# Scores of a fused attention kernel made four tiles ahead in one step, and what moves with them on VectorE and GpSimd

## The chip, the cores and the metric

The kernel runs on one core of a Trainium2 chip. The metric is device time in microseconds (us) of one execution. A core has five engines, each with its own list of instructions that it works through in order: TensorE (PE, matmuls; its weight loads are shown as PEld), VectorE (DVE), ScalarE (ACT), GpSimd (POOL) and SyncE (SP, which issues DMAs). They wait for one another by semaphores only.

## The reference

Three stages follow one another: attention that keeps the 32 largest scores of each row, a mixture of experts with a routing that runs along the sequence, and a Fourier mixer with a feed-forward part. The change lies in the first:

```python
scores = scale * np.matmul(q, k.transpose(0, 1, 3, 2))        # q, k, v: (4, 8, 576, 64)
kth = np.partition(scores, -top_k, axis=-1)[..., -top_k:-top_k + 1]   # top_k = 32
mask = scores >= kth
scores = np.where(mask, scores, -1000000000.0)
scores = scores - np.max(scores, axis=-1, keepdims=True)
attn = np.exp(scores)
attn = attn / (np.sum(attn, axis=-1, keepdims=True) + 1e-09)
return np.matmul(attn, v).astype(np.float32)
```

## The kernel before, in words

The attention is `attention()` (lines 280 to 955). Its rows of queries are cut into NTILE = 144 tiles of 128 rows; TPP = 9 tiles belong to one pair of heads. Each tile has 576 scores per row, held as two halves of SH = 288. Tiles are worked in pairs: pair c is tiles 2c and 2c+1, and there are 72 pairs. Every engine writes its list as a function `body(t)` called for t from -LQ to NTILE+3 (`run`, line 444); what one tile needs is spread over several values of t, called steps here.

TensorE, step t (line 578): four matmuls on the identity that compute nothing (`keep_clock`, line 493, only for t below EARLY0 = 83; they wait until ScalarE has taken the rows of tile t-2); `turn(t)`, five transposes of the masked exponentials, which wait for GpSimd's mask of tile t; `between(t, 0)`; `scores` of one half of a pair (an even step makes the first half of pair t+6, the odd step after it makes the second half); `between(t, 1)`; `values(t-1)`, ten instructions that multiply with v; `between(t, 2)`; and once in nine steps `gates(t)`. `between` holds work of later stages: hops of the early routing at steps 74 to 80 (HOPS, line 288), and from step 83 on the units of the early experts, 106 units over 60 steps, mostly one at place 0 and, in three steps of four, one at place 1 (`early_h`, `early_y`, `early_x`, lines 178 to 215).

PSUM has two banks for scores, ps_s[0] and ps_s[1], one for each tile of a pair, and only 288 of their columns are used: a first half must be evicted before the second is written, and a second half stays there until VectorE has read it (`pe.wait_ge(s_upper, k)`, line 477).

ScalarE, step t (line 629): in an even step `sign` of tiles t and t+1 (line 607, waits for VectorE's `under`, the threshold from the pair's 32nd value); `exp(t+2)` (line 618); the evictions of the transposes of tile t (lines 640, 642); `evict_scores` (line 621: two copies of 288 columns, one half of both tiles of a pair; for a first half it waits until GpSimd has masked the tile six before, since s_sb has NS = 6 buffers); the rows of tile t-1 (lines 654, 655, wait for `values(t-1)`); then gates and early experts.

GpSimd, step t (line 714): in an even step `sums` of pair t/2+2 (line 702, two additions, wait for both halves to be evicted); the mask of tile t (line 736, waits for sign and exp); in an odd step `lowers` of pair (t-1)/2+2 (line 712, two subtractions, wait for VectorE's `upper`). At steps 75 to 79 it also normalises rows, two tiles a step (line 442).

VectorE walks pair after pair through a list of 22 operations (`top_op`, line 761): 20 MAX8 and MATCH_REPLACE8 in the order of PLAN, over the larger ("upper") and the smaller ("lower") of each two scores, and two scans. Between them: after operations 4 and 5 of pair c, `upper` of the two tiles of pair c+1 (line 755, reads the first half in s_sb and the second half in PSUM, waits for the copy of the second half); after operations 1, 2, 3 the three small operations that give `under` for pair c-1 (`below_kth`, lines 792 to 798); from pair 38 on, two operations of the early routing after each (they await TensorE's hops at places given by AWAIT, line 289). Operations 0 and 1 of a pair need its `upper`, 2 and 3 need GpSimd's `lowers`.

The order around the change is this written-out list of steps; no planner is involved. In step t = 2c-2 ScalarE signs pair c-1 while VectorE is in pair c.

Of the kernel before, what the change touches and what calls it, by code (L numbers as in the profile page):

```python
# [29 lines left out]
NTILE = NPAIR * TPP  # L30
# [249 lines left out]
def attention(nc, env, q_h, k_h, v_h, vt_h):  # L280
# [1 line left out]


    ident, X, gd, lg = env["ident"], env["X"], env["gd"], env["lg"]
    LQ, LE = 6, 2
    MIDDLE = NTILE // 2
    ROUTE, NORM = MIDDLE // 2 + 2, MIDDLE + 3
    HOPS = [(MIDDLE + n, at) for n, at in ((2, 2), (3, 2), (4, 1), (4, 2), (5, 2), (8, 0))]
# [7 lines left out]
    with ExitStack() as ctx:  # L296
# [158 lines left out]
        def _(pe):  # L455
# [120 lines left out]
                        early_y(pe, env, j, m)  # L576

            def body(t):
                if live(t):
                    if t == 0:  # L580
                        pe.wait_ge(env["s_ident"], 1)
                    if 0 < t < EARLY0:
                        keep_clock(t, 4)
                    turn(t)
                between(t, 0)
                k = t + LQ
                if live(k):
                    scores(k - k % 2, k % 2)
                between(t, 1)
                if live(t - 1):  # L590
                    values(t - 1)
                between(t, 2)
                if gates_at(t):
                    gates(t)
# [5 lines left out]
        @block.scalar  # L600
        def _(act):
            act.dma_start(k_sb[0][:, :], k_h[0]).then_inc(s_qk_in[0], 16)

            def sign(k):
                act.wait_ge(s_under, 3 * (k // 2) + 3)
                act.wait_ge(s_exp, k + 1)
                act.activation(s_sb[k % NS][:, :], s_sb[k % NS][:, :], ACT.Sign, bias=under[:, (k // 2) % 2, k % 2:k % 2 + 1],  # L607
                               scale=1.0).then_inc(s_sign, 1)

            def exp(k):  # L610
                c, y = k // 2, k % 2
                if y == 0:
                    act.wait_ge(s_top, STEPS * c + 2)
                    act.activation(nmax[:, c % 2, :], top[c % 2][:, :, 0], ACT.Copy, scale=-SCALE).then_inc(s_nm, 1)
                if k >= NE:
                    act.wait_ge(s_tr, 2 * (k - NE + 1))
                act.wait_ge(s_nm, c + 1)
                act.activation(e_sb[k % NE][:, :], s_sb[k % NS][:, :], ACT.Exp, bias=nmax[:, c % 2, y:y + 1],  # L618
                               scale=SCALE).then_inc(s_exp, 1)

            def evict_scores(k):
                base, h = k - k % 2, k % 2
                for n in (base, base + 1):
                    act.wait_ge(s_qk, 2 * base + 2 * h + n - base + 1)
                    if h == 0 and n >= NS:
                        act.wait_ge(s_mask, n - NS + 1)
                    act.activation(s_sb[n % NS][:, h * SH:(h + 1) * SH], ps_s[n % 2][:, 0:SH], ACT.Copy).then_inc(s_copy, 1)  # L627

            def body(t):
                if live(t) and t % 2 == 0 and t < NTILE - 2:  # L630
                    sign(t)
                    sign(t + 1)
                if live(t + LE):
                    exp(t + LE)
                if live(t):
                    pair = eT[t % NT_]
                    act.wait_ge(s_tr, 2 * t + 1)
                    if t >= NT_:
                        act.wait_ge(s_pv, t - NT_ + 1)
                    act.activation(pair[:, 0:KC, :].rearrange("p c q -> p (c q)"), ps_t[:, :], ACT.Relu).then_inc(s_ev, 1)  # L640
                    act.wait_ge(s_tr, 2 * t + 2)
                    act.activation(pair[0:S - KC * P, KC, :], ps_o[t % 2][0:S - KC * P, 384:384 + P], ACT.Relu).then_inc(s_ev, 1)
                if live(t + LQ):
                    evict_scores(t + LQ)
                k = t - 1
                if live(k):
                    u, rt = k // TPP, ORDER[k % TPP]
                    act.wait_ge(s_pv, k + 1)
                    for two in range(2):
                        if (two == 0 and rt > MID) or (two == 1 and rt < MID):  # L650
                            continue
                        rows = slice(0, P) if rt != MID else slice(two * HALF, two * HALF + HALF)
                        c0 = two * VW
                        act.activation(gd[rows, rt, u, :], ps_o[k % 2][rows, c0 + D:c0 + VW], ACT.Copy)
                        op = act.activation(X[rows, rt, u * D:(u + 1) * D], ps_o[k % 2][rows, c0:c0 + D], ACT.Copy)  # L655
                    op.then_inc(s_o, 1)
                if gates_at(t):
                    u = (t + 2) // TPP
                    g = v_sb[u % 2][:, :, :].rearrange("p c (w x) -> p c w x", w=2)[:, :, :, D:D + E + 1]
                    src = ps_o[t % 2][:, GATES:GATES + 2 * (KC + 1) * (E + 1)].rearrange("p (c w e) -> p c w e", w=2, e=E + 1)  # L660
                    act.wait_ge(s_vw, u + 1)
                    act.activation(g[:, 0:KC], src[:, 0:KC], ACT.Copy).then_inc(s_vg, 1)
                    act.activation(g[0:S - KC * P, KC], src[0:S - KC * P, KC], ACT.Copy).then_inc(s_vg, 1)
                if t == HOPS[0][0] + 1:
                    act.wait_ge(r["s_sh"], 1)
                    act.activation(r["ex"][:, :, :], r["sh"][:, :, :], ACT.Exp).then_inc(r["s_ex"], 1)
                for kind, j, m in units_at(t):
                    if kind == "x":
                        early_x_out(act, env, j)
                    elif kind == "h" and m % (NF // 2) == NF // 2 - 1:  # L670
                        early_h_out(act, env, j, m // (NF // 2))
                    elif kind == "y" and m == NF - 1:
                        early_y_out(act, env, j)

            run(body)

        @block.gpsimd
        def _(pool):
# [35 lines left out]
            def body(t):  # L714
# [14 lines left out]
                    if t == unit_tile(("y", j, NF - 1)) + 4:  # L729
                        early_scatter(pool, env, j)  # L730
                if t % 2 == 0:
                    sums(t // 2 + 2)
                if live(t) and t < NTILE - 2:
                    pool.wait_ge(s_exp, t + 1)
                    pool.wait_ge(s_sign, t + 1)
                    pool.tensor_tensor(e_sb[t % NE][:, :], e_sb[t % NE][:, :], s_sb[t % NS][:, :], ALU.mult).then_inc(s_mask, 1)  # L736
                if t % 2 == 1:
                    lowers(t // 2 + 2)

            pool.memset(r["carry"][:, 0:1], 0.0).then_inc(r["s_zero"], 1)  # L740
            pool.memset(a["endb"][:, 0:1], 0.0).then_inc(a["s_end"], 1)
# [4 lines left out]
        def _(dve):  # L746
            then = chained(dve, s_a, [0])

            PLAN = [(step, y, low) for step in range(3) for low in range(2) for y in range(2)]
            PLAN += [(step, y, 0) for step in range(3, 7) for y in range(2)]  # L750

            def upper(k):

# [7 lines left out]
            def top_op(c, n):  # L761

                if n < 20:
# [6 lines left out]
                        else:  # L770
                            dve.wait_ge(s_split, 4 * c - 1 + y)
                    if step > 0:
                        dve.wait_ge(s_top, STEPS * c + (n - 3 if step < 4 else n - 1))
                    half = w_sb[(2 * c + y) % NW][:, low * SH:(low + 1) * SH]
                    first = 8 * (step // 2)
                    eight = ps_l[:, c % 2, y, 1 + first:9 + first] if low else top[c % 2][:, y, first:first + 8]
# [143 lines left out]
            for c in range(NTILE // 2):  # L920
                for n in range(STEPS):
                    top_op(c, n)
                    now[0] = (c, n)
                    if n in (4, 5) and c + 1 < NTILE // 2:
                        upper(2 * c + n - 2).then_inc(s_upper, 1)
                    if c > 0 and n in (1, 2, 3):
                        below_kth(c - 1, n - 1)
                    if c >= ROUTE:
# [1401 lines left out]
```

## Time and profile before

| | us |
|---|---|
| median of 3 runs | 1653.99 (1650.48 to 1660.36) |
| the profiled execution's own time | 1653.34 |
| its span from the first to the last instruction | 1651.5 |
| TensorE busy in the span | 1451.8 (88%) |
| VectorE busy | 996.8 (60%) |
| ScalarE busy | 686.9 (42%) |
| GpSimd busy | 540.3 (33%) |
| mean granted TensorE clock | 0.918 |

Times in the rows are microseconds from the span's start. A busy time that overlaps its neighbour comes from pipelining: what counts in a chain is the distance between starts. The granted clock is 1.00 at 2.4 GHz and 0.50 at 1.2 GHz; a mean between them is a mixture of the two. The attention ends near 901 us; what follows (routing, experts, mixer) is not touched by the change.

### The profile page before, as it was taken

What the parts mean: (1) busy time and instruction counts of PE and PEld (TensorE: products, weight loads), DVE (VectorE), ACT (ScalarE), POOL (GpSimd) and SP (SyncE); (2) the same over time, 40 slices, a digit from 0 to 9 for tenths busy, and PEclk for the clock granted to TensorE, in tenths of its full rate; (3) what the DMA queues carried; (4) which work ended last, traced back from release to release, by engine and by line L of the source; (5) the groups of instructions that cost most, each with busy time, mean ns of one, the idle gap of its engine ahead of it and who ended that gap; (6) DMA issues with size and microseconds to landing.
All of it is one profiled execution on the core that took longest, in us unless ns stands there. A gap on an engine that the chain in (4) does not pass through costs nothing. (4 is left out here: it accounts for less than half of the span.)

```text
span 1651.5 us, 24985 instructions
## 1 busy us (share of the span) xinstructions
PE 1451.8 (88%) x8088; PEld 1166.5 (71%) x8088; DVE 996.8 (60%) x3223; ACT 686.9 (42%) x1688; POOL 540.3 (33%) x617
## 2 busy tenths in 40 slices
PE   5888888888877778777877899999999999999998
PEld 3666666666666465554655699998677789889987
DVE  7778788878886665666666754445766332432222
ACT  4556566656444444554444344433422221321110
POOL 3545555555544443444443122121212110000001
PEclk9889899989777787888877999999999999999999
DMA  3101111010143222322221547644332111221111
GB/s 106 30 23 31 30 31 30 9 31 23 59 141 141 81 86 78 108 82 81 86 88 58 197 155 278 238 167 150 117 119 72 58 48 39 96 96 39 39 39 58
DMA packets 76567, 141.90 MB, mean 86 GB/s; under 512 B 27083, under 2 KB 27212, under 8 KB 76442
## 3 DMA queue, kind: packets, MB, share of 16 engines
q1 hardware_dynamic: 57994, 88.43, 16.0%
q10 hardware_dynamic: 11120, 29.66, 5.0%
q0 software_dynamic: 7328, 22.28, 3.8%
q8 instruction: 62, 1.02, 0.2%
q14 instruction: 63, 0.52, 0.1%
HBM read 116.75 MB, written 24.65 MB: 86 GB/s over the span
## 5 line engine op out<-in xcount | busy, mean ns | idle before, releaser
L517 PEld LDWEIGHTS ps_o<-v_sb,eT 128*128 128x128 f32 (+1 forms) x1440 | 203.7, 206 | 66.2 <-issue 28.6
L485 PE MATMUL ps_t<-ident,e_sb 128*128 128x128 f32 x576 | 110.2, 323 | 143.0 <-POOL e_sb L736 138.2
L702 POOL TENSOR_TENSOR w_sb<-s_sb 128x288 int32<-128x288 int32 x142 | 109.7, 793 | 383.3 <-ACT s_sb L627 379.9
L778 DVE MAX8 top<-w_sb 128x8 f32<-128x288 f32 x576 | 232.9, 444 | 0.2
L517 PE MATMUL ps_o<-v_sb,eT 128*128 128x74 f32 (+3 forms) x1440 | 229.6, 301 | 0.0
L736 POOL TENSOR_TENSOR e_sb<-e_sb,s_sb 128x576 f32<-128x576 f32 x142 | 197.3, 1409 | 77.9 <-ACT s_sb L607 77.8
L2041 DVE SCALAR_TENSOR_TENSOR h_lo<-ps_ch,h_hi 128x384 fp32r<-128x384 f32 x96 | 53.4, 556 | 235.0 <-ACT h_hi L1861 235.0
L755 DVE TENSOR_TENSOR w_sb<-s_sb,ps_s 128x288 f32<-128x288 f32 x144 | 64.6, 449 | 211.9 <-ACT s_sb L627 211.7
L780 DVE MATCH_REPLACE8 w_sb<-top,w_sb 128x288 f32<-128x288 f32 x432 | 188.9, 442 | 0.0
L485 PEld LDWEIGHTS ps_t<-ident,e_sb 128*128 128x128 f32 x576 | 75.0, 162 | 158.7 <-POOL e_sb L736 150.2
L1861 ACT ACTIVATE h_hi<-ps_ch 128x384 fp32r<-128x384 f32 x96 | 47.2, 492 | 279.8 <-PE ps_ch L1645 279.8
L627 ACT ACTIVATE s_sb<-ps_s 128x288 f32<-128x288 f32 x288 | 105.8, 408 | 108.5 <-PE ps_s L465 104.3
L465 PE MATMUL ps_s<-k_sb,q_sb 64*128 64x288 f32 x512 | 133.0, 549 | 10.5 <-DMA k_sb<-in_k 4.5
L1643 PE MATMUL ps_ch<-un_hi,w_hi 128*128 128x384 f32 x384 | 131.2, 342 | 1.6 <-DVE h_lo L2041 1.0
L640 ACT ACTIVATE eT<-ps_t 128x512 f32<-128x512 f32 x144 | 85.9, 597 | 110.2 <-PE ps_t L485 109.8
L1645 PE MATMUL ps_ch<-un_hi,w_lo 128*128 128x384 f32 x384 | 129.2, 337 | 0.0
L500 PE MATMUL ps_o<-ident 128*128 128x128 f32 x656 | 103.7, 306 | 28.8 <-ACT rows L655 28.8
L1644 PE MATMUL ps_ch<-un_lo,w_hi 128*128 128x384 f32 x384 | 128.8, 335 | 0.0
L778 DVE MAX8 ps_l<-w_sb 128x8 f32<-128x288 f32 x288 | 122.5, 455 | 5.7 <-POOL w_sb L712 5.2
L500 PEld LDWEIGHTS ps_o<-ident 128*128 128x128 f32 x656 | 87.1, 207 | 41.2 <-ACT rows L655 40.2
L618 ACT ACTIVATE e_sb<-s_sb,nmax 128x576 f32<-128x576 f32 x144 | 111.6, 775 | 8.9 <-issue 2.2
L1643 PE MATMUL ps_cy<-w_hi,h_hi 128*128 128x512 f32 x288 | 114.3, 397 | 0.0
(332 smaller groups left out, 2808.2 us busy)
## 6 DMA issues: line engine op xcount, KB each, us to landing
w<-in_w SPq DMA_DIRECT2D x18, 2048.0 KB, 13.2
w<-in_w ACTq DMA_DIRECT2D x14, 2048.0 KB, 8.3
stage<-in_w_ch SPq DMA_DIRECT2D x16, 512.0 KB, 5.9
q_sb<-in_q SPq DMA_DIRECT2D x16, 288.0 KB, 2.8
vT<-in_vt SPq DMA_DIRECT2D x16, 288.0 KB, 3.1
x_d<-rows SPq DMA_DIRECT2D x18, 256.0 KB, 2.9
x_d<-u POOLq DMA_DIRECT2D x18, 256.0 KB, 2.9
u<-x_d SPq DMA_DIRECT2D x18, 256.0 KB, 2.8
```

What stands on the lines that cost most here:

```text
L465: return pe.matmul(ps_s[k % 2][:, 0:SH], lhsT, k_sb[b][rows, h * SH:(h + 1) * SH], start=True, stop=True)
L485: mm = pe.transpose(ps_t[:, c * P:(c + 1) * P], e_sb[k % NE][:, c * P:(c + 1) * P], ident[:, :])
L500: pe.matmul(ps_o[k % 2][:, 384:384 + P], ident[:, :], ident[:, :], start=True, stop=True)
L517: mm = pe.matmul(ps_o[k % 2][:, lo:hi], eT[k % NT_][0:n, c, :], v_sb[b][0:n, c, lo:hi], start=(c == 0), stop=(c == KC))
L618: act.activation(e_sb[k % NE][:, :], s_sb[k % NS][:, :], ACT.Exp, bias=nmax[:, c % 2, y:y + 1], scale=SCALE).then_inc(s_exp, 1)
L702: pool.tensor_tensor(w[:, SH:S], x[:, 0:SH], x[:, SH:S], ALU.add).then_inc(s_split, 1)
L736: pool.tensor_tensor(e_sb[t % NE][:, :], e_sb[t % NE][:, :], s_sb[t % NS][:, :], ALU.mult).then_inc(s_mask, 1)
L778: dve.max(eight, half).then_inc(s_top, 1)
L780: dve.match_replace(out=half, in_to_replace=eight, in_values=half, imm_value=-BIG).then_inc(s_top, 1)
L1643: pe.matmul(out_, hi1, hi2, start=first, stop=False)
L1644: pe.matmul(out_, hi1, lo2, start=False, stop=False)
L1645: return pe.matmul(out_, lo1, hi2, start=False, stop=last)
```

## The change

LQ falls from 6 to 4. Both halves of pair t+4 are made in the even step t, ahead of `turn(t)`: the first half, then `between(t, 0)`, then the second. `between(t, 0)` now stands ahead of `turn(t)` in odd steps also. ScalarE evicts the first half ahead of the two signs and the second half behind them. VectorE's `upper` of the next pair moves from operations 4 and 5 to behind operation 17. On GpSimd `sums` moves from ahead of an even step's mask to behind the following odd step's mask, and `lowers` from behind an odd step's mask to ahead of the next even step's. PLAN is written in another form with the same order, and the wait inside it names the same operation as before.

```diff
-    LQ, LE = 6, 2
+    LQ, LE = 4, 2
...
             def body(t):
+                k = t + LQ
+                new = live(k) and k % 2 == 0
+                if new:
+                    scores(k, 0)
+                between(t, 0)
+                if new:
+                    scores(k, 1)
                 if live(t):
                     if t == 0:
                         pe.wait_ge(env["s_ident"], 1)
                     if 0 < t < EARLY0:
                         keep_clock(t, 4)
                     turn(t)
-                between(t, 0)
-                k = t + LQ
-                if live(k):
-                    scores(k - k % 2, k % 2)
                 between(t, 1)
                 if live(t - 1):
                     values(t - 1)
...
             def body(t):
+                new = live(t + LQ) and t % 2 == 0
+                if new:
+                    evict_scores(t + LQ)
                 if live(t) and t % 2 == 0 and t < NTILE - 2:
                     sign(t)
                     sign(t + 1)
+                if new:
+                    evict_scores(t + LQ + 1)
                 if live(t + LE):
                     exp(t + LE)
...
-                if live(t + LQ):
-                    evict_scores(t + LQ)
...
                 if t % 2 == 0:
-                    sums(t // 2 + 2)
+                    lowers(t // 2 + 1)
                 if live(t) and t < NTILE - 2:
...
                 if t % 2 == 1:
-                    lowers(t // 2 + 2)
+                    sums(t // 2 + 2)
...
-            PLAN = [(step, y, low) for step in range(3) for low in range(2) for y in range(2)]
-            PLAN += [(step, y, 0) for step in range(3, 7) for y in range(2)]
+            PLAN = [(step, y, low) for step, low in ((0, 0), (0, 1), (1, 0), (1, 1), (2, 0), (2, 1), (3, 0), (4, 0), (5, 0), (6, 0))
+                    for y in range(2)]
...
-                        dve.wait_ge(s_top, STEPS * c + (n - 3 if step < 4 else n - 1))
+                        dve.wait_ge(s_top, STEPS * c + PLAN.index((step - 1, y, low)) + 1)
...
-                    if n in (4, 5) and c + 1 < NTILE // 2:
-                        upper(2 * c + n - 2).then_inc(s_upper, 1)
+                    if n == 17 and c + 1 < NTILE // 2:
+                        for y in range(2):
+                            upper(2 * c + 2 + y).then_inc(s_upper, 1)
```

## Rows read from the trace of the kernel before

**Rows 1.** The page's part 5, costliest groups: busy, mean ns, idle before.

```profile
L778 DVE MAX8 top<-w_sb 128x8 f32<-128x288 f32 x576 | 232.9, 444 | 0.2
```

**Rows 2.** Stretches: line 614 (once a pair), clock, DMA; then PE, PEld, DVE, ACT, POOL.

```profile
14.58:409.06 394.48, 7.29 (x37) 0.94 0.10 28
409.06:488.14 79.08, 0.97 (x5) 0.72 0.24 81
488.14:900.51 412.37, 5.75 (x30) 0.81 0.27 94
...
14.58:409.06 394.48, 323.53 (x2032) 249.21 (x2032) 334.46 (x1305) 239.85 (x652) 214.76 (x223) 0.94 0.10 28
488.14:900.51 412.37, 326.49 (x1648) 233.74 (x1648) 265.35 (x1030) 198.29 (x538) 177.48 (x183) 0.81 0.27 94
```

**Rows 3.** Who waited for whom, 14 to 409 us, then 488 to 900: total, times, longest.

```profile
PE ps_t L485 <- POOL e_sb L736: 38.8, 35, 1.5
...
DVE w_sb L755 <- ACT s_sb L627: 139.2, 29, 8.7
PE ps_t L485 <- POOL e_sb L736: 84.2, 29, 3.8
```

**Rows 4.** Timeline of a plain pair: start us, us, engine, line, what, [idle before].

```profile
247.38 0.15 DVE L798 SCALAR_TENSOR_TENSOR under<-ulp,ps_l 128x2 f32<-128x2 f32 x1
...
248.70 1.48 PE L517 MATMUL ps_o<-v_sb,eT 128*128 128x74 f32 x10
...
249.24 0.45 DVE L755 TENSOR_TENSOR w_sb<-s_sb,ps_s 128x288 f32<-128x288 f32 x1 [1.29 <-ACT s_sb L627]
...
250.40 1.44 ACT L607 ACTIVATE s_sb<-s_sb,under 128x576 f32<-128x576 f32 x2
...
250.56 1.16 PE L500 MATMUL ps_o<-ident 128*128 128x128 f32 x8 [0.38 <-ACT rows L655]
...
251.32 2.78 POOL L736 TENSOR_TENSOR e_sb<-e_sb,s_sb 128x576 f32<-128x576 f32 x2 [0.18 <-ACT s_sb L607]
...
252.78 0.66 PE L485 MATMUL ps_t<-ident,e_sb 128*128 128x128 f32 x4 [1.06 <-POOL e_sb L736]
...
253.47 0.76 PE L465 MATMUL ps_s<-k_sb,q_sb 64*128 64x288 f32 x4
...
254.05 1.56 POOL L712 TENSOR_TENSOR w_sb<-w_sb 128x288 int32<-128x288 int32 x2
...
254.16 1.48 PE L517 MATMUL ps_o<-v_sb,eT 128*128 128x74 f32 x10
```

**Rows 5.** Timeline in the stretch with early experts, around the scores.

```profile
713.39 0.76 PE L465 MATMUL ps_s<-k_sb,q_sb 64*128 64x288 f32 x4
...
714.18 0.71 ACT L627 ACTIVATE s_sb<-ps_s 128x288 f32<-128x288 f32 x2 [0.65 <-PE ps_s L465]
...
718.75 1.02 PE L213 MATMUL ps_a<-w,stage 128*128 128x512 f32 x2
...
719.71 0.76 PE L465 MATMUL ps_s<-k_sb,q_sb 64*128 64x288 f32 x4
```

**Rows 6.** Timeline: a wait for the mask and what follows it.

```profile
705.67 0.86 PE L485 MATMUL ps_t<-ident,e_sb 128*128 128x128 f32 x4 [3.08 <-POOL e_sb L736]
...
706.54 1.91 PE L213 MATMUL ps_a<-w,stage 128*128 128x512 f32 x2
```

**Rows 7.** Timeline: the pair after an odd step with gates, about 355 us.

```profile
355.55 1.12 PE L485 MATMUL ps_t<-ident,e_sb 128*128 128x128 f32 x4 [1.51 <-POOL e_sb L736]
...
358.07 2.62 PE L517 MATMUL ps_o<-v_sb,eT 128*128 128x74 f32 x10
```

**Rows 8.** Timeline: the inverse of the early routing, step 80.

```profile
471.18 1.11 PE L485 MATMUL ps_t<-ident,e_sb 128*128 128x128 f32 x4 [6.30 <-POOL e_sb L736]
...
472.30 3.87 PE L550 MATMUL ps_a<-early_what,early_at_pos 128*128 128x21 f32 x18
...
476.20 0.17 DVE L897 COPY early_tok<-ps_a 128x7 f32<-128x7 f32 x1 [3.54 <-PE ps_a L550]
```

## The prediction

> **What bounds the kernel now.** I read the page's groups first, then the attention by stretch. The line that runs once a pair gives the pace [rows 2]: 37 pairs in 394.48 us (10.66 each) up to 409 us, 5 pairs in 79.08 while the early routing runs, 30 in 412.37 with early experts (the last of the 30 stands at the very end, so 29 periods of 14.2). VectorE is busy 334 of 394 us in the first stretch, but only 265 of 412 in the third, and it waits there 139.2 us for ScalarE's copy of scores [rows 3]. So it is not the bound; it is late because the copies are. TensorE waits once a pair for GpSimd's mask: 38.8 us over 35 waits in the first stretch, 84.2 over 29 in the third, 2.9 us each [rows 3].
>
> The timeline of a plain pair shows a loop through four engines [rows 4]. Values start at 248.70 and last 1.48. Groups of matmuls overlap by 0.07 (scores from 253.47 last 0.76, values start at 254.16), so the next could start at 250.11; I call that point V. ScalarE takes the tile's rows and starts the signs at 250.40, V+0.29; the mask starts 0.92 later, at 251.32; half of its 2.78 us on, the turn starts at 252.78, V+2.67. TensorE then does two whole steps before the next V. The `under` that the signs also need ended at 247.53, 2.87 us before they began: VectorE is not in this loop. The loop is 9.64 us long here, of which TensorE serves 7 and stands in the hole between V and the turn, with only the clock keepers in it [rows 4]. In the third stretch no clock keepers are there and the hole is empty.
>
> **The change part by part.**
>
> (a) Scores leave the steps. From the turn at 252.78 scores start 0.69 later and values 0.69 after that [rows 4]. Without scores behind the turn, values follow it directly: 0.69 us less in each of two steps, 1.37 in a pair. The scores now lie in the hole.
>
> (b) The first half's copies now stand ahead of the signs. Copies start 0.79 us after the scores do (713.39 to 714.18) and two take 0.71 [rows 5]. Scores start at V at the earliest, so the signs start at V+0.79+0.71 = V+1.50 and not at V+0.29: 1.21 us more in the loop; mask and turn follow with the old distances, turn at V+3.88. The lower bound of this cost is 0.71 (copies alone, scores already there), which only a late V could give; the upper is 1.21 plus 0.4, about what lies between V and the clock keepers at 250.56 [rows 4]. I take 1.21.
>
> (c) Does the rest fit the hole? The second half needs both copies, V+1.55; then 0.69 of scores and 1.16 of clock keepers (their rows were taken before the signs started) end at V+3.4, ahead of V+3.88. It fits, by 0.5.
>
> (d) First stretch: 1.21 - 1.37 = -0.16 us a pair, 37 pairs: -6 us. Bounds: -0.66 a pair (cost 0.71), +0.24 (cost 1.61), so -24 to +9.
>
> (e) `between(t, 0)` ahead of the turn. In an even step its unit, 0.96 us by start distance (718.75 to 719.71) [rows 5], moves into the hole between the two halves, where TensorE would wait for the copies anyway: V to 0.69 first half, unit to 1.65, second half to 2.4, turn at 3.88. In an odd step it only changes places with the turn, since that mask was ready. Third stretch: 1.21 - 1.37 - 0.96 = -1.12 a pair, for 29 periods -32 us. ScalarE's early evictions at the end of an odd step used to delay the signs; they now run while it waits for the first half. I count nothing for it.
>
> (f) TensorE's clock. The granted clock is 0.94 in the first stretch and 0.81 in the third [rows 2], so (1 less the mean, over 0.5) about 12% and 38% of the time at 1.2 GHz. Where it is low, ten values matmuls take 2.62 us (358.07) and not 1.48, 1.77 times as long [rows 7, 4]. The time it costs is the low share times the busy share times (1 - 1/1.77 = 0.43): 412 x 0.38 x 0.79 x 0.43 = 53 us in the third stretch, 394 x 0.12 x 0.82 x 0.43 = 17 in the first. What TensorE did before: it stood 3.08 us, then the unit that takes 1.02 elsewhere took 1.91 [rows 6, 5]; likewise after gates, whose matmuls are tiny, and a wait of 1.51 [rows 7]. With waits of 1.1 us the first stretch had 0.94, with waits of 2.9 the third had 0.81 [rows 2, 3]. The new wait of the third stretch is 3.88 - 2.4 = 1.5 us, near the first. I take 0.94 for it: 0.38 falls to 0.12, 53 falls to about 15, -38 us. In the first stretch the gates of an odd step are now followed at once by scores, so I count half of its 17 as gone, -8. Bounds: nothing won (0), and all won (-70).
>
> The rule that speaks against this: standing and transposes now lie in one piece, 1.5 us and 0.7, with thin values behind them instead of scores. The Trainium skill, TensorE: Matmul & The Clock Gate, Part 4: PE-mode transpose, says that transposes do not count as busy in the way matmuls do. By it the low clock would stay, the -38 and -8 would be 0, and the sum would end near 1607. The trace does not settle it: in each pair so far matmuls stand close behind the transposes.
>
> (g) VectorE's `upper` behind operation 17. It waits for the second half's copies, which follow two signs (1.44): V+2.94 to V+3.65. VectorE frees itself 8.35 us after the last time (9.64 less the 1.29 it waited [rows 4]), so it can keep any period above that. The wait of 139.2 us goes; nobody behind it was waiting, so it is worth nothing by itself. What is late next is operation 2, which needs `lowers`. GpSimd: masks V+2.42 to 5.20, sums (two, taken as long as lowers, 1.56) to 6.8, lowers to 8.35. VectorE gets from `upper` to operation 2 over two MATCH_REPLACE8, two scans and two MAX8, some 2.5 us (0.44 each at most by [rows 1], less for the scans), and comes to it between V+6.9 and 8.2: it waits for 1.5 us at most. `under` is then ready near V+9.0, and the next signs start at 9.48 + 1.50 = V+10.98: cover of 2 us. Cost 0; without the cover 1 us a pair.
>
> (h) GpSimd's moves cost nothing else: `sums` waits for copies of V+3.65 and its place comes at 5.20. No DMA is moved; SyncE's loads of q and k wait for the count of scores and come a step or two later against steps 7 or more ahead of use: 0.
>
> (i) Middle stretch. VectorE is the bound there. At step 80 the inverse ran behind the turn for 3.87 us, and VectorE waited 3.54 us for it, although TensorE had stood 6.30 us just before [rows 8]. As `between(80, 0)` it now runs ahead of the turn, in that wait: -3.5. Hops come earlier by the scores left out, and `upper` no longer waits: about -4 more. I take -8, bounds 0 and -12.
>
> Sum: (d) -6, (e) -32, (f) -38 and -8, (i) -8, together -92. The profiled execution's own time is 1653.34 (span 1651.5), 0.65 below the median; 1653.3 - 92 = 1561, and I say 1560.
>
> **Rivals.** Half of the clock gain (0.12) or none (0.08). The loop shortens as worked out, but the clock stays low because what follows the turn is thin. For it: standing, transposes and thin values now lie in one piece. Against it: 0.94 in the first stretch, where each pair also has a wait. By the rule named under (f) none is the case to expect. None gives 1653 - 6 - 32 - 8 = 1607, half 1584.
>
> Still faster (0.13): the clock is hardly low anywhere (-60 of 70), and the middle gives its bound: 1653 - 6 - 32 - 60 - 12 = 1543; with (d) at half its bound 1537.
>
> No change (0.03): signs wait for scores by more than 1.21. TensorE's first half waits for `upper` of the pair before; if VectorE comes to it after V, everything waits. For it: VectorE is the fullest engine of the first stretch. Against it: operation 3 is done near V+8.8, fourteen more of at most 0.44 and two uppers of 0.45 bring it to V+15.9, which is 6.4 us behind the next V (9.48) and 3 us ahead of the one where it is needed. The delay must eat 92 / 71 = 1.3 us a pair: 1653 within 8.
>
> Slower (0.05): operation 2 of VectorE's list. `lowers` is now made between `upper` and that operation, behind two masks and sums. It decides once GpSimd is later than 2 us behind V+8.35, so that `under` comes after V+10.98; each microsecond beyond is a microsecond of every pair. With 1 us beyond in 37 pairs (+37), and with the clock of the third stretch now for the longer standing (394 x 0.38 x 0.82 x 0.43 = 53, less 17: +36), the first stretch gives +73 - 6, the third still -32: 1688. Against it: GpSimd is idle for 180 of the 394 us [rows 2].
>
> That the change does not do what it says is not likely: PLAN keeps its order, and nothing else could take scores back.
>
> **How the numbers follow.** Forecast 0.59, as the likeliest: 1560, its own range 1545 to 1580. The rivals on the faster side reach 1537 and 1607. From 1532 to 1610 leaves out the no-change and slower cases (0.08) and some 0.1 at the ends. A measurement of this kernel can tell about 0.5% (8 us) from no change. Faster 0.92, same 0.03, slower 0.05.
>
> **What would show it.** In the changed profile: values directly behind the turn, start distance 0.69; copies of the first half 0.8 us behind V and signs right behind them; turn at V+3.9; a plain pair of the first stretch of 9.5 us; of the third stretch near 11.8 in the mean; PE's wait for the mask near 0.6 and 1.5 us; the granted clock of the third stretch at 0.94 or so; the wait of `upper` for copies nearly gone, and a new wait of MAX8 for `lowers`, 30 to 70 us in all; the inverse ahead of turn 80. I am wrong if the clock stays near 0.81, or if ScalarE's signs wait for `under`.

## The result, and the profile after

The changed kernel takes 1474.24 us (median of 4 runs, 1469.77 to 1475.78) against 1654.11 for the kernel before: a ratio of 0.8905, 95% interval 0.887 to 0.8939. I had said 1560, within 1532 to 1610. The way was right, the size was not: 180 us went and not 92. The profiled execution's span fell from 1651.5 to 1474.0, by 178 us; the tables below take that one apart.

The page of the changed kernel, parts 1 and 2:

```profile
span 1474.0 us, 24985 instructions
...
PE 1349.2 (92%) x8088; PEld 1116.1 (76%) x8088; DVE 995.9 (68%) x3223; ACT 679.4 (46%) x1688; POOL 541.9 (37%) x617
...
PEclk9999999999789989999989999999999999999999
```

The work on VectorE, ScalarE and GpSimd is what it was. TensorE has as many instructions, but is busy for 103 us less: most of that is the clock, which is at 90% or more in all but four of the 40 slices now. The same stretches as in [rows 2], by the line that runs once a pair (us; PE, PEld, DVE, ACT, POOL busy; clock; DMA):

```profile
14.68:357.91 343.23, 290.21 (x2030) 235.43 (x2030) 334.02 (x1302) 235.35 (x653) 214.44 (x221) 0.99 0.11 32
357.91:423.89 65.98, 56.59 (x315) 45.48 (x314) 61.25 (x235) 33.08 (x93) 40.41 (x42) 0.77 0.30 99
423.89:728.08 304.19, 267.66 (x1650) 202.21 (x1650) 262.71 (x1017) 195.96 (x537) 178.89 (x185) 0.96 0.36 126
```

| stretch | before | after | difference | predicted |
|---|---|---|---|---|
| first, 37 pairs | 394.5 | 343.2 | -51.2 | -14 |
| middle, 5 pairs | 79.1 | 66.0 | -13.1 | -8 |
| third, 29 periods | 412.4 | 304.2 | -108.2 | -70 |
| behind the attention | 751.0 | 745.9 | -5.1 | 0 |

The clock of the first stretch rose from 0.94 to 0.99, of the third from 0.81 to 0.96. The waits, for the first stretch and then for the third, against [rows 3]:

```profile
PE ps_s L465 <- ACT s_sb L630: 26.8, 37, 0.9
...
PE ps_t L485 <- POOL e_sb L742: 9.7, 25, 0.7
...
DVE ps_l L784 <- POOL w_sb L718: 8.8, 26, 0.9
```

```profile
DVE ps_l L784 <- POOL w_sb L718: 35.7, 39, 3.9
PE ps_t L485 <- POOL e_sb L742: 33.5, 29, 1.5
PEld ps_s L465 <- ACT s_sb L630: 13.1, 18, 1.5
...
DVE w_sb L761 <- ACT s_sb L630: 5.2, 5, 2.0
```

VectorE's wait for copies went from 139.2 to 5.2 us. TensorE waits 33.5 us for masks in the third stretch and not 84.2. New, as foreseen, is MAX8 waiting for GpSimd's `lowers`, 8.8 and 35.7 us; it moves nothing, for the signs wait for `under` only once in each of the two stretches, by 0.4 and 0.6 us. A plain pair of the first stretch, against [rows 4]:

```profile
210.04 0.60 PE L485 MATMUL ps_t<-ident,e_sb 128*128 128x128 f32 x4
...
210.59 1.38 PE L517 MATMUL ps_o<-v_sb,eT 128*128 128x74 f32 x10
...
212.35 1.16 PE L500 MATMUL ps_o<-ident 128*128 128x128 f32 x8 [0.38 <-ACT rows L661]
...
213.35 0.60 PE L485 MATMUL ps_t<-ident,e_sb 128*128 128x128 f32 x4
...
213.90 1.27 PE L517 MATMUL ps_o<-v_sb,eT 128*128 128x74 f32 x9
...
214.84 0.51 PE L465 MATMUL ps_s<-k_sb,q_sb 64*128 64x288 f32 x1
...
215.00 0.27 PE L517 MATMUL ps_o<-v_sb,eT 64*128 64x74 f32 x1
...
215.63 0.71 ACT L630 ACTIVATE s_sb<-ps_s 128x288 f32<-128x288 f32 x2
...
216.23 1.44 ACT L610 ACTIVATE s_sb<-s_sb,under 128x576 f32<-128x576 f32 x2
216.39 0.76 PE L465 MATMUL ps_s<-k_sb,q_sb 64*128 64x288 f32 x4 [0.58 <-ACT s_sb L630]
217.08 1.16 PE L500 MATMUL ps_o<-ident 128*128 128x128 f32 x8
217.15 2.78 POOL L742 TENSOR_TENSOR e_sb<-e_sb,s_sb 128x576 f32<-128x576 f32 x2 [2.73 <-ACT s_sb L610]
...
218.61 0.66 PE L485 MATMUL ps_t<-ident,e_sb 128*128 128x128 f32 x4 [0.37 <-POOL e_sb L742]
```

The loop can be read off the starts: turn to values 0.55, to keepers 1.76, to the odd turn 1.00, to values 0.55, to the first score 0.94, to the copies 0.79, to the signs 0.60, to the mask 0.92, to the next turn 1.46: 8.57 us, where 9.64 stood before. I had worked out 9.48. (Counted from one execution of the line that runs once a pair to the next, the same pair takes 8.68 us.) Three distances are not as foreseen. Values follow the turn by 0.55 and not by 0.69. The signs follow the start of the copies by 0.60 and not by 0.71. And the first score starts at 214.84, before the last values matmul at 215.00, 0.94 behind the start of the values, where I had put V at 1.41.

Not every pair is that short. In the first stretch the lengths repeat every nine pairs (18 tiles, two pairs of heads) to within 0.02 us, but for the first two pairs and a few longer ones. At full clock a round of nine took 91.9 us before (9.64 to 10.87 a pair) and takes 83.1 now (8.68 to 10.20): 0.98 us less a pair, or 36 us in 37 pairs. The long pairs took the rest: before, four of them (13.98 to 15.35 us, at a clock of 0.59 to 0.64) hold 17 us more than the same pairs at full clock; now 2.4 us are left of that.

### The profile page after: what moved, and what is told of

Same layout as the page of the kernel before. It is cut to its first block and busy times, and to the rows that moved or that the text cites. A ratio compares the mean times of both kernels' runs of the same rounds, so it can differ in the third digit from the quotient of the medians.

```text
span 1474.0 us, 24985 instructions
## 1 busy us (share of the span) xinstructions
PE 1349.2 (92%) x8088; PEld 1116.1 (76%) x8088; DVE 995.9 (68%) x3223; ACT 679.4 (46%) x1688; POOL 541.9 (37%) x617
## 5 line engine op out<-in xcount | busy, mean ns | idle before, releaser
L517 PEld LDWEIGHTS ps_o<-v_sb,eT 128*128 128x128 f32 (+1 forms) x1440 | 192.0, 196 | 23.8 <-issue 12.5
L517 PE MATMUL ps_o<-v_sb,eT 128*128 128x74 f32 (+3 forms) x1440 | 209.1, 284 | 0.0
L465 PE MATMUL ps_s<-k_sb,q_sb 64*128 64x288 f32 x512 | 124.2, 474 | 43.3 <-ACT s_sb L630 32.0
L485 PE MATMUL ps_t<-ident,e_sb 128*128 128x128 f32 x576 | 95.8, 292 | 48.3 <-POOL e_sb L742 46.9
L485 PEld LDWEIGHTS ps_t<-ident,e_sb 128*128 128x128 f32 x576 | 69.6, 148 | 76.0 <-POOL e_sb L742 65.7
L718 POOL TENSOR_TENSOR w_sb<-w_sb 128x288 int32<-128x288 int32 x142 | 110.0, 797 | 19.6 <-DVE w_sb L761 11.5
L648 ACT ACTIVATE eT<-ps_t 128x512 f32<-128x512 f32 x144 | 85.9, 596 | 65.6 <-PE ps_t L485 60.6
L465 PEld LDWEIGHTS ps_s<-k_sb,q_sb 64*128 64x128 f32 x512 | 54.5, 194 | 80.2 <-ACT s_sb L630 59.5
```

What stands on the lines that cost most here:

```text
L465: return pe.matmul(ps_s[k % 2][:, 0:SH], lhsT, k_sb[b][rows, h * SH:(h + 1) * SH], start=True, stop=True)
L485: mm = pe.transpose(ps_t[:, c * P:(c + 1) * P], e_sb[k % NE][:, c * P:(c + 1) * P], ident[:, :])
L517: mm = pe.matmul(ps_o[k % 2][:, lo:hi], eT[k % NT_][0:n, c, :], v_sb[b][0:n, c, lo:hi], start=(c == 0), stop=(c == KC))
L718: pool.tensor_tensor(w[:, SH:S], w[:, SH:S], w[:, 0:SH], ALU.subtract).then_inc(s_split, 1)
```

## The experiments

The theory after the result had three parts: the loop is shorter than worked out because the scores start beside the last values; the low clock cost more than I had counted; and what stands in the hole between V and the turn decides the clock. The rivals: earlier weight loads, the shorter loop alone, or VectorE's new place. All ratios below are to the kernel before on the same chip.

| run | median us | ratio (95% interval) | first stretch, clock | third stretch, clock |
|---|---|---|---|---|
| e1 | 1507.1 | 0.9124 (0.9087 to 0.9161) | 364.5, 0.98 | 303.2, 0.99 |
| e2 | 1528.5 | 0.924 (0.9195 to 0.9285) | 350.9, 0.97 | 347.6, 0.88 |
| e3 | 1583.3 | 0.9594 (0.953 to 0.9658) | 388.4, 0.96 | 346.8, 1.00 |
| e4 | 1582.8 | 0.9564 (0.9517 to 0.9612) | 418.7, 0.85 | 330.4, 0.91 |
| e5 | 1609.9 | 0.9723 (0.9684 to 0.9761) | 394.8, 0.94 | 367.9, 0.86 |
| e6 | 1445.1 | 0.8723 (0.8693 to 0.8753) | 342.1, 0.98 | 271.6, 1.00 |
| e7 | 1461.2 | 0.883 (0.8798 to 0.8862) | 331.9, 0.95 | 296.6, 0.98 |
| e8 | 1470.0 | 0.8872 (0.8847 to 0.8898) | 345.4, 0.98 | 293.5, 1.00 |
| e9 | 1447.3 | 0.8757 (0.8723 to 0.8791) | 342.9, 0.89 | 272.5, 0.99 |
| e10 | 1463.4 | 0.8851 (0.8818 to 0.8883) | 363.2, 0.83 | 272.1, 1.00 |
| e11 | 1449.6 | 0.8785 (0.8735 to 0.8835) | 345.3, 0.88 | 272.0, 1.00 |
| e12 | 1433.1 | 0.8659 (0.8628 to 0.8689) | 330.4, 0.99 | 275.9, 0.97 |

How much of a stretch is chance can be seen where two kernels have the same list: the first stretch took 394.5, 388.4 and 394.8 us in the kernel before, e3 and e5, and 343.2, 350.9 and 345.4 in the changed kernel, e2 and e8, at clocks from 0.94 to 0.96 and from 0.97 to 0.99. Differences of a whole first or third stretch below 8 us are not read. Pair by pair one can read more: e3 differs from the kernel before by over 0.02 us in only three of the 37 pairs (by 0.4, 2.1 and 4.3), so what differs is how often the clock was low. The middle stretch is steadier (79.1 in both the kernel before and e3, 66.0 in both the changed kernel and e8). Behind the attention the kernel before, e3 and e5 took 751.0, 752.0 and 748.7 us.

**e1, the short chunk of the values first** (on the changed kernel)

```diff
-                for c in range(KC + 1):
+                for c in (KC, 0, 1, 2, 3):
...
-                                   start=(c == 0), stop=(c == KC))
+                                   start=(c == KC), stop=(c == 3))
```

> The changed kernel, but values() takes its chunk of 64 rows first and its four chunks of 128 rows after it, so that a full-height matmul and not a half-height one stands right ahead of the first scores. In the changed kernel's trace the first score starts at 214.84, beside the last (64-row) chunk of the values that started at 213.90: 0.94 us after their start, where I had counted 1.41. Theory (scores run beside the half-height chunk, and that is why the copies ahead of the signs cost 0.6 and not 1.2): the scores start 1.3 to 1.4 us after the values, signs and turn 0.3 to 0.45 us later, a plain pair of the first stretch takes 9.0 to 9.1 us and not 8.68, and the whole 72 pairs cost 20 to 30 us more: 1494 to 1504 us. Rival (the scores are early because their weights are loaded early, whatever stands ahead): the start distance stays near 0.95 and the time stays at 1474 within 5.

The timeline of e1 in a plain pair:

```profile
223.01 1.48 PE L517 MATMUL ps_o<-v_sb,eT 64*128 64x74 f32 x10
...
224.42 0.76 PE L465 MATMUL ps_s<-k_sb,q_sb 64*128 64x288 f32 x4
...
225.21 0.71 ACT L630 ACTIVATE s_sb<-ps_s 128x288 f32<-128x288 f32 x2 [0.39 <-PE ps_s L465]
```

With a chunk of 128 rows ahead of them, the scores start 1.41 us behind the values, 0.47 later than with the chunk of 64 rows: the rival falls. The short chunk behind the turn costs another 0.28 a pair: the values start 0.64 behind the turn and not 0.55, in both steps, and the keepers 1.87 behind the values and not 1.76. Together 0.75, which is what this pair is longer (9.43 and not 8.68). Others are 0.5 longer; a round of nine takes 87.5 us and not 83.1, 0.49 a pair, which is 18 of the 21 us by which the first stretch grew. The whole, 1507.1, lies 3 us above the theory's range.

The changed kernel also shows what the early start needs. In four pairs of its first stretch the first score uses 128 rows, and there it starts 1.32 us behind the values, as it does in e1:

```profile
204.44 1.38 PE L517 MATMUL ps_o<-v_sb,eT 128*128 128x74 f32 x10
...
205.76 0.75 PE L465 MATMUL ps_s<-k_sb,q_mid 128*128 128x288 f32 x2
```

The third stretch as a whole did not grow (303.2 at clock 0.99, against 304.2 at 0.96), but its pairs did: 24 of 29 are longer, by 7.1 us together or 0.30 each, and the other five are shorter by 8.1. Those five are pairs that e8 shortens too, that is, pairs that low clock had lengthened in the changed kernel. The profiled execution of e1 was its fastest by 9 us, and some 13 of the 33 us between the medians lie in executions of which there is no trace.

**e2, `between(t, 0)` behind the turn again** (on the changed kernel)

```diff
                 if new:
                     scores(k, 0)
-                between(t, 0)
-                if new:
                     scores(k, 1)
...
                     turn(t)
+                between(t, 0)
                 between(t, 1)
```

> The changed kernel with between(t, 0) put back behind turn(t) in all steps; scores, copies, upper, sums and lowers stay as changed. Theory (the early experts' unit in the hole is worth its 0.96 us in each pair of the third stretch, and fills the hole so that the clock stays high): third stretch longer by 28 us for the unit and some 10 to 20 for a clock that falls from 0.96 to about 0.90, the inverse of step 80 again behind its turn, 3 us: 1510 to 1525 us. Rival (the unit's place is of no account, all comes from scores leaving the steps): 1474 within 6, clock 0.96.

Third stretch +43 us at a clock of 0.88, middle +4: the theory, though 1528.5 lies 3 us above its range. The first stretch has the same list and a round of nine of 83.0 us as in the changed kernel; its +8 are long pairs and no effect of the edit. The unit alone is 29 x 0.96 = 28 us, so the clock is worth some 15.

**e3, fillers in the hole of the kernel before**

```diff
                     if 0 < t < EARLY0:
                         keep_clock(t, 4)
+                    elif t >= EARLY0 and t % 2 == 0:
+                        keep_clock(t, 8)
```

> The kernel before, with eight matmuls on the identity (they compute nothing that is used) ahead of the turn of each even step from step 83 on, in the hole where TensorE waits 2.9 us for the mask. The order of scores, copies and between() is the old one. Theory (a good half of what the third stretch gained is the granted clock, which falls after a wait in which TensorE stands): clock of 488 to 900 us rises from 0.81 to 0.93 or more, that stretch falls by 35 to 50 us, the whole to 1605 to 1620. Rival (the clock follows from elsewhere, the stretch gained by its shorter loop alone): clock near 0.81, time 1654 or up to 20 more for the fillers.

Useless matmuls took the kernel's time to 0.9594. Stretches one and three of e3, columns as above:

```profile
14.77:403.19 388.42, 316.94 (x2032) 244.35 (x2032) 334.59 (x1305) 239.76 (x653) 214.67 (x223) 0.96 0.10 28
482.30:829.11 346.81, 319.23 (x2106) 246.19 (x2107) 263.08 (x1022) 197.54 (x537) 177.59 (x183) 1.00 0.32 111
```

The third stretch fell by 65.6 us at a clock of 1.00, more than theory (35 to 50) and prediction (53) said; the order of the work is the old one. So the low clock cost at least 65.6 us there. It cost more only if the useless matmuls lengthen pairs, and there is no sign of that: the four pairs that are no shorter in e3 (10.11, 12.73, 13.02 and 13.04 us before) are longer by 0.01 at most.

**e4, `upper` behind operations 4 and 5 again** (on the changed kernel)

```diff
-                    if n == 17 and c + 1 < NTILE // 2:
-                        for y in range(2):
-                            upper(2 * c + 2 + y).then_inc(s_upper, 1)
+                    if n in (4, 5) and c + 1 < NTILE // 2:
+                        upper(2 * c + n - 2).then_inc(s_upper, 1)
```

> The changed kernel with VectorE's two upper operations put back behind operations 4 and 5 of its list; all else stays as changed. Theory (with scores made four ahead the second half is copied behind two signs that themselves wait for operation 3, so the place behind 17 is what makes the lead of four possible): VectorE stands 2 us or more in each pair for the copies, a loop under, signs, copies, upper of VectorE's 8.3 us and 2.3 of waiting bounds all pairs near 10.7 us: first stretch about 395 us and not 343, the whole 1530 to 1560. Rival (VectorE has so much slack that the place does not matter): 1474 within 8.

The timeline of e4 shows the ring from `under` over signs and copies to `upper`:

```profile
361.52 0.15 DVE L804 SCALAR_TENSOR_TENSOR under<-ulp,ps_l 128x2 f32<-128x2 f32 x1
361.70 1.44 ACT L610 ACTIVATE s_sb<-s_sb,under 128x576 f32<-128x576 f32 x2 [1.55 <-DVE under L804]
...
363.47 0.45 DVE L761 TENSOR_TENSOR w_sb<-s_sb,ps_s 128x288 f32<-128x288 f32 x1 [1.38 <-ACT s_sb L630]
...
364.08 0.44 PE L485 MATMUL ps_t<-ident,e_sb 128*128 128x128 f32 x2 [2.03 <-POOL e_sb L742]
```

Signs wait 1.55 us for `under`, VectorE 1.38 for the copies, and a pair takes 10.36 us. It came out slower than the 1530 to 1560 expected: TensorE now waits 2.03 us and its clock fell to 0.85 in the first stretch, where 37 pairs of 10.37 us make 384 of the 418.7 and the other 35 us lie in longer pairs, of up to 15 us. Without VectorE's part 1582.8 - 1474.2 = 108.6 of the 179.9 us won are lost, 60%: it is the condition of the rest, though it shortens no loop that bound before.

**e5, `between(t, 0)` ahead of the turn, alone** (on the kernel before)

```diff
             def body(t):
+                between(t, 0)
                 if live(t):
...
                     turn(t)
-                between(t, 0)
```

> The kernel before with one thing of the change alone: between(t, 0) ahead of turn(t) in all steps; scores stay behind the turn, six ahead, and the clock keepers where they are. Theory (of the 108 us that the third stretch gained, a unit moved into the hole is worth 28 by its length, and as much again by the clock, since TensorE stands 1.6 and not 2.9 us): third stretch of 345 to 370 us and not 412, its clock at 0.90 or more, VectorE's 3.5 us at step 80 gone: 1585 to 1610 us in all. Rival (only with scores in the hole does the clock hold): clock stays near 0.81, third stretch 380 to 390, 1620 to 1630.

Third stretch 367.9 us at 0.86, 44 less than before, and the middle 75.6, 3.5 less; the median lies at the upper end of the theory's range. The clock gained less than I had expected (0.90).

**e6, the first half's copies between the signs** (on the changed kernel)

```diff
-                if new:
-                    evict_scores(t + LQ)
                 if live(t) and t % 2 == 0 and t < NTILE - 2:
                     sign(t)
+                if new:
+                    evict_scores(t + LQ)
+                if live(t) and t % 2 == 0 and t < NTILE - 2:
                     sign(t + 1)
```

> The changed kernel with ScalarE's copies of the first half behind the first of the two signs and not ahead of it. Theory (signs now start 0.99 us behind V because they stand behind copies that wait for scores; V is where the values' matmuls end): the first sign and its mask come 0.7 us earlier. In the first stretch the second half of the scores and the clock keepers then end after the mask, at V+3.4, so a plain pair stays near 8.68; in the third stretch, where no keepers stand, turns come 0.5 to 0.7 us earlier: 15 to 20 us less in all, 1452 to 1462. Rival (TensorE's own work in the hole already ends last, or VectorE's list): 1474 within 6.

Better than expected: 0.8723, third stretch 33 us shorter, clock 1.00. The first stretch stays, because the keepers end last; its timeline (the mask of one tile lasts 1.39, so it was done at 219.86):

```profile
217.55 0.78 ACT L610 ACTIVATE s_sb<-s_sb,under 128x576 f32<-128x576 f32 x1
218.22 0.71 ACT L630 ACTIVATE s_sb<-ps_s 128x288 f32<-128x288 f32 x2
218.47 2.79 POOL L743 TENSOR_TENSOR e_sb<-e_sb,s_sb 128x576 f32<-128x576 f32 x2 [3.35 <-ACT s_sb L610]
...
218.98 0.76 PE L465 MATMUL ps_s<-k_sb,q_sb 64*128 64x288 f32 x4 [1.11 <-ACT s_sb L630]
219.66 1.16 PE L500 MATMUL ps_o<-ident 128*128 128x128 f32 x8
...
220.66 0.60 PE L485 MATMUL ps_t<-ident,e_sb 128*128 128x128 f32 x4
```

**e7, clock keepers in even steps alone** (on the changed kernel)

```diff
-                    if 0 < t < EARLY0:
+                    if 0 < t < EARLY0 and t % 2 == 0:
```

> The changed kernel with the four clock keepers of the first stretch in even steps alone. Theory (they fill a hole in even steps, but in odd steps they stand in the loop with their 1.0 us, and VectorE's list of 8.35 us is next): a plain pair falls from 8.68 to 8.4, 10 us in the stretch, if the clock holds near 0.97: 1462 to 1470. Rival (the odd step's keepers are what holds the clock): the clock of the first stretch falls to 0.90 or less, which costs more than the loop gains: 1475 to 1500.

The theory, a little below its range of 1462 to 1470: first stretch 331.9 at 0.95. A pair in it takes 8.9 us, not 8.4, and its signs wait for `under`, so VectorE is next:

```profile
291.29 1.45 ACT L610 ACTIVATE s_sb<-s_sb,under 128x576 f32<-128x576 f32 x2 [1.01 <-DVE under L804]
```

**e8, clock keepers in the third stretch also** (on the changed kernel)

```diff
-                    if 0 < t < EARLY0:
+                    if 0 < t < EARLY0 or t % 2 == 0 and t > 0:
```

> The changed kernel with four clock keepers also in the even steps of the third stretch, where TensorE still waits 33.5 us in 29 waits for the mask. Theory (what is left of the low clock there, 0.96, costs 304 x 0.08 x 0.43 = 10 us, and the keepers fit into the wait): clock 0.99 or 1.00, the stretch 5 to 10 us shorter, 1464 to 1470 in all. Rival (1.0 us of keepers is longer than what is left of many waits, of 0.5 to 1.5 us, and lies in the loop): the clock rises but the time does not fall, or rises by up to 10.

The third stretch of e8, columns as above:

```profile
426.10:719.55 293.45, 283.59 (x1880) 219.50 (x1881) 262.57 (x1017) 196.62 (x537) 179.16 (x185) 1.00 0.38 131
```

Third stretch 293.5 at 1.00, 10.7 less: six pairs are shorter by 12.4 together, five longer by 0.2 to 0.4, the others the same within 0.02. By the whole time alone the gain would not be seen (0.8872 and 0.8905, with intervals that overlap). Together with e3 this parts the third stretch: at full clock 346.8 before and 293.5 after, so 53 us are the shorter loop, so far as the useless matmuls cost both kernels the same; the low clock took 65.6 before and still takes 10.7 after, so 55 us are the clock.

**e9, e10, e11: e6 with fewer keepers.** e9 has the four in even steps alone (the diff), e10 in odd steps alone (`t % 2 == 1` in its place), e11 two in each step (`keep_clock(t, 2)` under the old condition):

```diff
-                    if 0 < t < EARLY0:
-                        keep_clock(t, 4)
+                    if 0 < t < EARLY0 and t % 2 == 0:
+                        keep_clock(t, 4)
```

> Copies of the first half between the two signs (as in e6) and the four clock keepers of the first stretch in even steps alone (as in e7). If the two gains add: first stretch as e7's 332 us, third as e6's 272: 1430 to 1440. In e6 TensorE came to the turn 0.8 us after the mask was done, with keepers last, so that in the first stretch a unit of work less should show fully unless VectorE's list ends last; rival: VectorE (8.4 to 8.9 us a pair, ScalarE's signs waited for under in e7) takes over at once, first stretch 330 or more, 1440 and above.

> As e9, but the four keepers stand in odd steps alone. The same number of matmuls is left out, now from the piece between V and the even turn. If only the loop's length counts, as e9, 1430 to 1440; if the clock depends on what stands next to the waits, the clock of the first stretch is lower than e9's (0.93 or less) and the time 5 to 15 us longer, 1440 to 1455.

> As e6, with two clock keepers and not four in each step of the first stretch. Half a microsecond leaves each step: a plain pair of 8.6 should fall to VectorE's 8.4 at most, 5 to 10 us in the stretch, clock 0.95 to 0.98: 1435 to 1442. Rival: clock below 0.93, no gain against 1445.

The gains do not add. The clock of the first stretch falls to 0.89, 0.83 and 0.88, though single pairs are as short as 7.3 to 7.9 us; the stretch takes 343, 363 and 345 us, no better than e6's 342. Of the expectations, the rival of e11 foresaw this; the second branch of e10 foresaw the lower clock, but not as much of it (1463.4 and not 1440 to 1455). e9 lies in the range of its rival, but that put it down to VectorE and not to the clock. Leaving keepers out of even steps is dearest. Those stand next to the waits, which is a likely reason; e10 against e9 shows the price of the place, not why.

**e12, the keepers between the two halves** (on e6; none left out)

```diff
                 between(t, 0)
+                if 0 < t < EARLY0:
+                    keep_clock(t, 4)
                 if new:
                     scores(k, 1)
...
-                    if 0 < t < EARLY0:
-                        keep_clock(t, 4)
                     turn(t)
```

> As e6, with the four clock keepers of the first stretch moved between the two halves of the scores, where TensorE waits 1.1 us for the copies; none is left out. In e6 the keepers ended 0.8 us after the mask was done and held the turn. Theory (place, not number, is what they cost): the turn comes 0.5 to 0.8 us earlier, a plain pair falls from 8.65 to 8.4 or less, where VectorE ends last, the clock stays at 0.97 or more: first stretch 325 to 335 us and not 342, the whole 1430 to 1438. Rival (VectorE or GpSimd ends last already): 1445 within 5.

The fastest of all: 1433.1 us, 0.8659 (0.8628 to 0.8689). Its first stretch takes 330.4 us at 0.99, 11.7 less than e6's; 7 of these come from the round of nine (80.0 us and not 81.7), the rest from single long pairs. The timeline shows the keepers in the wait for the copies, and the signs now behind VectorE:

```profile
243.93 1.16 PE L500 MATMUL ps_o<-ident 128*128 128x128 f32 x8
244.12 0.15 DVE L805 SCALAR_TENSOR_TENSOR under<-ulp,ps_l 128x2 f32<-128x2 f32 x1
244.30 0.78 ACT L610 ACTIVATE s_sb<-s_sb,under 128x576 f32<-128x576 f32 x1 [0.50 <-DVE under L805]
...
245.73 0.76 PE L465 MATMUL ps_s<-k_sb,q_sb 64*128 64x288 f32 x4 [0.64 <-ACT s_sb L630]
...
246.69 0.55 PE L485 MATMUL ps_t<-ident,e_sb 128*128 128x128 f32 x3 [0.20 <-POOL e_sb L743]
```

## Why the prediction was wrong in size

The mechanism stood: scores out of the steps and into the hole, the clock up, VectorE no bound. What failed are sizes: the price of the copies ahead of the signs (b), what two steps save (a), and the low clock (f). The 178 us of the profiled executions, by the experiments and the lengths of pairs:

| us | predicted | measured |
|---|---|---|
| first stretch, loop | -6 | -36 |
| first stretch, clock | -8 | -15 |
| middle | -8 | -13 |
| third stretch, loop | -32 | -53 |
| third stretch, clock | -38 | -55 |
| behind the attention | 0 | -5 |

**(a) and (b), the loop.** I put -0.16 us on a plain pair; it came to -0.96 (9.64 to 8.68), and to -0.98 in the mean of nine. The step that failed is "scores start at V at the earliest". They start 0.47 earlier, beside the last chunk of the values, which has 64 rows as the scores have; e1 took that away and got the 0.47 back. The signs also follow the start of the copies by 0.60 and not by 0.71. So the price of copies ahead of signs was 0.63 (values to signs 1.70 before, 2.33 after) and not 1.21. And two steps without scores gave 1.61 and not 1.37, since the values stand 0.55 behind the turn without scores between. With the keepers 0.11 nearer that is 1.61 + 0.11 - 0.63 = 1.09 from turn to turn (9.64 to 8.57). The Trainium skill, TensorE: Matmul & The Clock Gate, Part 3: Packing small matmuls, says that matmuls on different groups of rows can run beside one another. The trace agrees, so far as its records tell which score is which. By the kernel's code the short chunk uses rows 0 to 63. The score that starts early at 214.84 is the first tile's, on rows 64 to 127. In twelve other pairs up to 360 us the first tile's scores are on rows 0 to 63, and there the second tile's weight load, for rows 64 to 127, stands 0.20 ahead of the load that carries the first tile's wait. Where neither score is on rows 64 to 127 alone (128 rows, then rows 0 to 63), the 1.32 of 205.76 stands. My bound for this term (0.71 at the least) was passed as well.

**(e), the third stretch's loop.** -32 predicted, -53 at full clock (e3 against e8). The closer values would give 29 x 0.24 = 7 of the missing 21. The earlier scores would give 29 x 0.47 = 14, but e1 makes the pairs there longer by only 0.30, its own extra cost behind the turn included: 9 us at most. The rest, and ScalarE's early evictions for which I counted nothing, stay open.

**(f), the clock.** I multiplied the low share by TensorE's busy share, as if low clock and standing were spread alike: 53 us for the third stretch, where e3 measured 65.6. Without that factor the row gives 412 x 0.38 x 0.43 = 67, but this is no rule either. In the first stretch the four pairs at low clock cost 17 us, which is what I had with the factor (20 without it), and in e4 the low clock cost 35, where the factor gives 44 and its absence 54. So what a low share costs depends on the stretch; why it is most in the third was not tested. Of the 65.6 us there 55 were won, not 38; in the first stretch 15 of 17, not 8. The 5 behind the attention are little more than the 3 by which kernels with the same list differ there. That the clock follows what stands in the hole is shown by e3, e5, e8 and, the other way, by e4 and e9 to e11. The rival by the rule on transposes, that the clock stays low because standing and transposes lie in one piece, fell: 0.96. It does not show that transposes count.

**(c)** The second half and the keepers fitted into the hole: TensorE waited 0.37 us more for the mask (0.5 foreseen), and 0.58 for the copies.

**(g)** `upper` waits no longer and MAX8 waits for `lowers`, 8.8 and 35.7 us, near what was said; `under` was ready at 214.98, 1.25 us ahead of the signs: less cover than the 2 us I had, because the loop got shorter. The slower rival needed GpSimd beyond that cover; it did not come, but e7 and e12 use the cover up.

**(i)** Middle stretch -13 and not -8; the inverse ran ahead of the turn, and e2 and e5 price its place at 3.8 and 3.5 us (3.5 foreseen). What the other 9 us are was not tested.

**The range.** "Still faster" stopped at 1537 since the first stretch's loop was bounded by a term that was itself wrong, the third's had no faster bound at all, and the clock was bounded by 70 us. All these errors lay on the same side.

## What to carry to other kernels

Do not price a low TensorE clock from its mean: the same formula was right in one stretch (17 us), 13 us too low in another and 9 too high in a third case. Try it on the unchanged kernel: a few useless matmuls in the longest wait show what the clock is worth before anything is moved. Compare runs pair by pair where a program repeats itself: lengths agreed to 0.02 us, and chance stood apart in single long pairs, where whole stretches differ by up to 8 us. When work is moved into a wait, put first what another engine needs (the sign, e6) and last nothing that holds the next step (the keepers, e12); here this took 180 us of gain to 221. Read distances between starts again for the new neighbours: they depend on what stands next to each other, and 0.96 us a pair was 36 us in the first stretch.

## What the runs showed of the hardware that I had not expected

A matmul on rows 64 to 127 that follows one on rows 0 to 63 starts before that one is through: 0.94 us behind the start of the ten values matmuls when their short chunk is last, 1.41 when it is first (e1). It even starts ahead of matmuls that stand before it in TensorE's list (214.84 against 215.00 above), so that list is not worked through strictly in order. In the third stretch a clock of 0.81 against 1.00 was 65.6 of 412 us with the same work in the same order and useless matmuls added (e3). Kernels with the same list in a stretch of 345 us differed by up to 7.7 us there. And where the keepers stand matters beside how many there are: with half of them, 0.89 (even steps) and 0.83 (odd steps); with all of them 0.98.
